# A fused attention and two-layer MLP kernel on one core: the written-out orders of VectorE and ScalarE set anew, and six output tiles held back at the end

## The reference

```python
# q, k, v: 4 batches, 8 heads, 576 positions, head size 64, float32
pooled = softmax(mean4(q) @ mean4(k).T / 8) @ mean4(v)      # 144 positions, repeated 4 times
local  = softmax(where(|i - j| < 4, q @ k.T / 8, -1e9)) @ v
x = (repeat(pooled, 4) + local)                             # -> [2304 tokens, 512]
x = (sigmoid(x @ w_gate) * (x @ w_val)) @ w_out             # 512 -> 1536 -> 512
h = x @ w_in2;  out = (h * sigmoid(1.702 * h)) @ w_out2     # 512 -> 2048 -> 512
```

## Time and profile before

| | before |
|---|---|
| median of the runs | 888.92 us |
| profiled execution, its own time | 887.71 us |
| its span, first to last instruction | 886.0 us |
| TensorE busy, matmul | 863.6 us (97%) |
| VectorE busy | 639.4 us (72%) |
| GpSimd busy | 591.5 us (67%) |
| ScalarE busy | 486.2 us (55%) |
| granted TensorE clock | 1.00 over the whole span |
| DMA, mean | 208 GB/s |

### The profile page before, as it was taken

The page is one execution under the profiler, slowest core; times in us unless marked ns, Lnnn a source line. Parts: engine busy times, 40 slices in busy tenths (PEclk is TensorE's granted clock), DMA queues, the critical chain, the costliest instruction groups (busy, mean ns, idle before and its releaser), DMA issues.

```text
span 886.0 us, 18369 instructions
## 1 busy us (share of the span) xinstructions
PE 863.6 (97%) x6638; PEld 830.4 (94%) x6638; DVE 639.4 (72%) x1140; ACT 486.2 (55%) x1083; POOL 591.5 (67%) x471
## 2 busy tenths in 40 slices
PE   8999999999999999999999899999999999999997
PEld 6877899999999999899999899999999999999996
DVE  5767545555658575967575977878787878878777
ACT  5777754545436355545355555664566456555651
POOL 5688988988658639773639765864678645845541
PEclk9999999999999999999999999999999999999999
DMA  8877366686956796828596815425236750646422
GB/s 323 264 229 215 136 255 243 224 341 259 355 163 221 258 351 225 298 80 286 204 338 234 275 47 191 156 95 202 96 119 214 286 190 25 213 171 225 160 75 72
DMA packets 74778, 184.26 MB, mean 208 GB/s; under 512 B 5569, under 2 KB 31169, under 8 KB 71873
## 3 DMA queue, kind: packets, MB, share of 16 engines
q1 hardware_dynamic: 74688, 183.10, 59.0%
HBM read 141.66 MB, written 41.42 MB: 207 GB/s over the span
## 4 chain that ended last, share of the span: by engine, by line
PE 81%; issue 6%; DVE 5%; POOL 4%; ACT 2%; DMA 1%; SPq 1%; DVEq 0%; ACTq 0%; POOLq 0%
PE o_ps L788 9%; PE o_ps L790 9%; PE o_ps L789 9%; PE d_ps L642 6%; PE o_ps L633 6%; PE d_ps L644 5%; PE d_ps L643 5%; PE s_ps L642 5%; PE s_ps L644 5%; PE s_ps L643 5%; PE t_ps L642 3%; PE t_ps L644 3%; PE t_ps L643 3%; PE o_ps L606 1%; POOL v L2099 1%
## 5 line engine op out<-in xcount | busy, mean ns | idle before, releaser
L788 PE MATMUL o_ps<-g_hi,v 128*128 128x384 f32 x504 | 169.7, 337 | 5.4 <-DVE att L1752 2.7
L790 PE MATMUL o_ps<-g_hi,v 128*128 128x384 f32 x504 | 169.6, 337 | 0.0
L789 PE MATMUL o_ps<-g_lo,v 128*128 128x384 f32 x504 | 169.4, 336 | 0.0
L1752 DVE TENSOR_TENSOR att<-o_ps,att 128x384 f32<-128x384 f32 x212 | 117.2, 556 | 55.7 <-PE o_ps L790 54.3
L2099 POOL TENSOR_TENSOR v<-v_f,v 128x512 fp32r<-128x512 f32 x72 | 95.3, 1343 | 51.4 <-ACT v L1055 51.4
L642 PE MATMUL d_ps<-xs_hi,w 128*128 128x384 f32 x360 | 122.3, 340 | 5.9 <-DVE s_ps L1610 3.4
L2099 POOL TENSOR_TENSOR v<-raw,v 128x512 fp32r<-128x512 f32 x54 | 71.1, 1316 | 82.9 <-ACT v L1048 82.9
L644 PE MATMUL d_ps<-xs_hi,w 128*128 128x384 f32 x360 | 120.7, 335 | 0.0
L643 PE MATMUL d_ps<-xs_lo,w 128*128 128x384 f32 x360 | 120.6, 335 | 0.0
L642 PE MATMUL s_ps<-xs_hi,w 128*128 128x384 f32 x300 | 101.9, 340 | 2.8 <-POOL xs_lo L2129 2.3
L788 PEld LDWEIGHTS o_ps<-g_hi,v 128*128 128x128 f32 x504 | 94.7, 188 | 7.2 <-issue 4.2
(11 more groups left out here) (181 smaller groups left out, 2122.0 us busy)
## 6 DMA issues: line engine op xcount, KB each, us to landing
w<-w_split SPq DMA_DIRECT2D x48, 768.0 KB, 7.0
w<-w_split SPq DMA_DIRECT2D x48, 512.0 KB, 7.8
w<-w_split SPq DMA_DIRECT2D x96, 256.0 KB, 5.0
w_split<-w SPq DMA_DIRECT2D x12, 1792.0 KB, 6.8
raw<-in_w_out_dram SPq DMA_DIRECT2D x36, 512.0 KB, 4.5
w_split<-job_w SPq DMA_DIRECT2D x8, 1792.0 KB, 9.5
vw<-in_v_win_dram SPq DMA_DIRECT2D x16, 390.0 KB, 4.8
raw<-in_w_gate_val_dram SPq DMA_DIRECT2D x12, 512.0 KB, 3.9
```

The costliest lines, as they stand in the source:

```text
L788: pe.matmul(bank, vh, gh, start=(start and k == c), stop=False, skip_group_check=True)
L789: pe.matmul(bank, vh, gl, start=False, stop=False, skip_group_check=True)
L790: mm = pe.matmul(bank, vl, gh, start=False, stop=(k == c + 1), skip_group_check=True)
L1752: vec.tensor_tensor(part, value, part, ALU.add).then_inc(y_added, 1)
```

## The change

VectorE's and ScalarE's lists in the four functions are set anew: instructions move by a few places, none is added or dropped. On SP, one load moves behind a store and a load. On TensorE, six tiles of the pair before the last are held back instead of four, `second_pair(38, 4)` to `(38, 6)`. All saved gated values of the last two groups get places of their own in the ring of x (`end`), and gelu no longer waits there for the tiles that read `g_f`. GpSimd's list is as it was.

```diff
...
         job_w = {i: place(f"job_w{i}", [P, 2, NP, WG], F32R, at=at_x(i)) for i in (7, 4, 1)}
         job_f = {i: place(f"job_f{i}", [P, 2, NP, WG], at=at_x(i)) for i in (7, 4, 1)}
         job_raw = {i: place(f"job_raw{i}", [P, 4, WG], at=at_x(i) + 8 * NP * WG) for i in (7, 4, 1)}
-        end_11 = place("end_11", [P, NT], at=at_x(4))
-        end_21 = [place(f"end_21{i}", [P, NT], at=at_x(2 + i)) for i in range(2)]
+        end = place("end", [P, 2, 3, NT], at=at_x(2))
...
             return att[:, p, c * PASS + t * NT:c * PASS + (t + 1) * NT]
         def saved_11_at(k):
-            return g_f[k % 2][:, 0, T2, :] if k != NG - 2 else end_11[:, :]
+            return g_f[k % 2][:, 0, T2, :] if k < NG - 2 else end[:, k % 2, 0, :]
         def saved_12_at(k):
-            return g_f[k % 2][:, 1, T2, :]
+            return g_f[k % 2][:, 1, T2, :] if k < NG - 2 else end[:, k % 2, 1, :]
         def saved_21_at(k):
-            return g_f[k % 2][:, 0, T4, :] if k < NG - 2 else end_21[k % 2][:, :]
+            return g_f[k % 2][:, 0, T4, :] if k < NG - 2 else end[:, k % 2, 2, :]
         def gated_at(k, n, bank):
...
             for k in range(G1 - 1):
                 if k >= 1 and k + 1 < G1:
                     load_out(k + 1)
-                load_in(LAST[k + 1] + 2)
                 if k == 2:
                     store_job(0)
                     load_job(1)
+                load_in(LAST[k + 1] + 2)
                 if k == 4:
                     store_job(1)
                 if k < G1 - 2:
...
                 p3(FIRST[c])
                 head(FIRST[c + 1])
                 step(FIRST[c + 2])
-                for i in range(NP if c + 4 < NG else NP - 2):
+                for i in range(NP if c + 4 < NG else NP - 3):
                     second_pair(c, i)
             c = NG - 2
             p4(FIRST[c])
             p3(FIRST[c])
             head(FIRST[c + 1])
-            second_pair(c - 2, NP - 2)
+            second_pair(c - 2, NP - 3)
             p3(FIRST[c + 1])
             p4(FIRST[c + 1])
+            second_pair(c - 2, NP - 2)
             second_pair(c - 2, NP - 1)
             for i in range(NP):
                 second_pair(c, i)
...
                 sigmoid(k, 12, z_bank)
             def gelu(k, n, bank):
-                if n in SLOT and (n != 21 or k < NG - 2) and (n != 11 or k != NG - 2):
+                if n in SLOT and k < NG - 2:
                     act.wait_ge(y_ready, g_free(k, SLOT[n]))
                 nc.scalar.activation(gated_at(k, n, bank), bank[FIRST[k] % 2], ACT.Gelu_apprx_sigmoid).then_inc(gated[n], 1)
...
                 n, m = FIRST[k + 1], LAST[k + 1]
                 snap_p1(n)
                 hi22(k)
-                hi21(k)
                 if k == 5:
                     round_t1(1)
-                sig11(k + 1)
                 if k == 5:
                     round_t3(1)
+                sig11(k + 1)
+                hi21(k)
                 snap_u2(n)
                 hi12(k)
+                snap_u3(n)
                 if m < MADE:
                     round_in(m)
                     round_in_sums(m)
-                snap_u3(n)
                 if k == 5:
                     round_t4(1)
                     round_b22(1)
...
                 if k in (1, 3):
                     job_a(k // 2)
                     job_s(k // 2)
+                sig12(k + 1)
+                snap_p1(m)
                 if k == 4:
                     round_b11(1)
                     round_b21(1)
-                sig12(k + 1)
-                snap_p1(m)
                 if FIRST[k + 2] < MADE:
                     round_in(FIRST[k + 2])
                 snap_u2(m)
-                hi11(k + 1)
                 if FIRST[k + 2] < MADE:
                     round_in_sums(FIRST[k + 2])
+                hi11(k + 1)
                 snap_u3(m)
                 if k == 4:
                     round_t2(1)
...
                 if last:
                     round_b11(q + 1)
                 snap_u2(FIRST[d])
+                if c in (G1 + 2, G1 + 6, G1 + 8):
+                    job_a({2: 3, 6: 5, 8: 6}[c - G1])
                 hi_t1(c)
                 sig11(d)
+                if last:
+                    round_b21(q + 1)
                 if c == G1:
                     v_s1(c)
                 snap_u3(FIRST[d])
                 hi_t3(c)
-                if c in (G1 + 2, G1 + 6, G1 + 8):
-                    job_a({2: 3, 6: 5, 8: 6}[c - G1])
                 snap_p1(LAST[d])
                 hi_t2(c)
-                if last:
-                    round_b21(q + 1)
                 sig22(d)
                 sig21(d)
                 hi_t4(c)
...
                 if c == G1:
                     job_a(2)
                 snap_u3(LAST[d])
+                snap_p1(FIRST[n])
                 if last:
                     round_t1(q + 1)
-                snap_p1(FIRST[n])
                 hi22(d)
                 if last:
                     round_t3(q + 1)
                 hi21(d)
+                snap_u2(FIRST[n])
+                hi_t1(d)
+                hi_t3(d)
                 if c == G1:
                     job_s(2)
-                snap_u2(FIRST[n])
-                hi_t1(d)
-                snap_u3(FIRST[n])
-                hi_t3(d)
                 hi_t2(d)
                 v_a12(n)
                 hi_t4(d)
                 if last:
                     round_t4(q + 1)
                     round_b22(q + 1)
+                snap_u3(FIRST[n])
                 if c in (G1 + 2, G1 + 8):
                     job_a({2: 4, 8: 7}[c - G1])
-                v_a11(n)
                 if c in (G1 + 2, G1 + 8):
                     job_s({2: 4, 8: 7}[c - G1])
+                v_a11(n)
                 if layer(n) == 1:
                     sig11(n)
                     sig22(n)
...
                 if not late:
                     v_s2(c)
                     v_s4(c)
-                gelu11(d)
                 snap_u2(FIRST[d])
                 hi_t1(c)
                 hi_t3(c)
+                gelu11(d)
                 hi11(d)
                 snap_u3(FIRST[d])
                 hi_t2(c)
+                snap_p1(FIRST[n])
                 if last:
                     round_t1(q + 1)
                 elif late:
...
                 else:
                     v_s3(c)
                     v_a22(c)
-                snap_p1(FIRST[n])
-                hi_t4(c)
                 if last:
                     round_t3(q + 1)
                 gelu22(d)
+                hi_t4(c)
                 gelu21(d)
+                hi21(d)
                 if last:
                     snap_u2(FIRST[n])
-                hi21(d)
                 gelu12(d)
                 if not last:
                     snap_u2(FIRST[n])
...
                 hi_t2(d)
                 if not late:
                     v_a12(n)
+                if first and q + 1 < len(PHASES):
+                    round_b11(q + 1)
+                    round_b21(q + 1)
                 if c == START[q] + 2 and q + 1 < len(PHASES):
                     round_t2(q + 1)
                 hi_t4(d)
-                if first and q + 1 < len(PHASES):
-                    round_b11(q + 1)
-                    round_b21(q + 1)
                 gelu11(n)
                 if last:
                     round_t4(q + 1)
                     round_b22(q + 1)
                 if late:
                     v_a12(n)
+                hi11(n)
                 v_a11(n)
-                hi11(n)
                 gelu22(n)
                 hi22(n)
...
                 d = c + 1
                 gelu21(c)
                 hi21(c)
+                snap_p1(FIRST[d])
                 gelu12(c)
-                snap_p1(FIRST[d])
+                hi_t1(c)
+                snap_u2(FIRST[d])
                 v_s1(c)
-                v_s2(c)
-                v_s4(c)
                 gelu11(d)
-                snap_u2(FIRST[d])
-                hi_t1(c)
                 hi11(d)
                 snap_u3(FIRST[d])
                 gelu22(d)
-                hi_t3(c)
-                v_s3(c)
+                hi22(d)
+                v_s2(c)
                 gelu12(d)
-                hi_t2(c)
                 gelu21(d)
                 hi21(d)
-                hi22(d)
+                v_s4(c)
+                hi_t1(d)
+                hi_t3(c)
+                hi_t3(d)
+                hi_t2(c)
+                hi_t2(d)
+                v_s3(c)
+                hi_t4(c)
                 v_a22(c)
-                hi_t1(d)
-                hi_t4(c)
-                hi_t3(d)
-                hi_t2(d)
                 hi_t4(d)
             act.wait_ge(zeroed, 1)
...
                     low11(c)
                     c22(LAST[c])
                 gate22(c)
+                low22(c)
                 gate21(c)
                 c12(LAST[c])
                 gate12(c)
-                low22(c)
                 make_t1(c)
                 c11(FIRST[d])
                 make_t3(c)
...
```

(59 more changed lines are left out.)

## The result

The changed kernel takes 872.29 us (median of 5 runs, 871.56 to 873.14) against 888.92 (886.49 to 890.87): ratio 0.9821, 95% interval 0.9808 to 0.9834. Forecast were 878.9 and a range of 873.5 to 885.5.

The account below looks back on a forecast made before the run. TensorE's stream was taken to bound the kernel, with only its holes to win. Terms summed to 12.5 us, less 2.5 for new waits: 887.71 - 10.0 = 877.7, plus 1.2 to the median: 878.9; range 873.5 to 885.5.

Parts of the forecast that it names:

- deduction: Over the 18 pairs: 2.5 us taken off the summed gain for some ten new small waits of 0.25 us.
- f: First pair of the next second-layer pass, twice: c22 ahead of low11 removes a wait; 1.5 us gain (0.5 to 2.0).
- Term b: First-layer pairs: low22(c) ahead of gate21(c), job_s(2) behind a snapshot; 0.8 us gain (-0.5 to 1.1).
- a: Entry into the second pass: round_t1 and round_t3 earlier, so GpSimd's chain starts sooner; 0.9 us gain (0 to 1.2).
- c: Ends of first-layer passes, twice: low21(d) earlier, round_t1 later so x_t3 can start first; 3.0 us gain (0 to 4.6).
- Term g: The kernel's end: six tiles held back and values kept apart, p4 of the last pair earlier; 3.3 us gain (1.5 to 4.3).
- e: Last pair of a second-layer pass, twice: x_t3 and round_t3 earlier; 1.2 us gain (-0.6 to 1.9).
- Term d: Second-layer pairs: c22 ahead of low_t2 and low11, gelu11 and hi11 behind hi_t3; 1.8 us gain (-2 to 2.6).
- more: Rival: x_t3 starts first at both passes, no new waits; 872.7 us, 873.9 as a median; chance 0.15.
- Only the end and f: Rival: elsewhere small waits only change places, meeting GpSimd anew; 882.9 us, 884.1 as a median; chance 0.17.
- The slower one: Rival: in layer one's first pass a circle of waits costs five blocks 2.5 us each; median 891.4; chance 0.05.
- such a circle: Layer one, first pass: TensorE's p7, snapshot, round_in, low_in, low_in_sums, TensorE's p6; if closed, 12.5 us lost in all.

Follow-up runs that it names:

- the end with c22: Kernel before with six tiles held back at the end and c22 ahead of low11 in the second layer's pairs: 881.77 us, ratio 0.9929.
- pair_of_one alone: Kernel before with only pair_of_one's two instruction lists (first layer's pairs) set anew: 882.49 us, ratio 0.9923.

## Why the prediction was wrong

The reading of the profile held: only TensorE's holes could be won, and the terms are all there with their sign. The miss is 6.6 us, in these steps.

**The deduction failed: "I take off 2.5, some ten new ones of 0.25".** The new waits did come, and in about that size: followed product by product, TensorE loses 0.1 to 0.4 us at nine places in the trace of the change, 2.6 in all (two of them, 0.32 each, f had counted with 0.25). One of them:

```profile
356.57 0.41 PE L641 MATMUL s_ps<-xs_hi,w 128*128 128x384 f32 x1 [0.18 <-ACT snap L1104]
```

But what went is 18.6 us, where the terms had 12.5, and among it are small waits of before that no term had named, such as those at p7 at 318.25, 408.82 and 452.90 us (0.25 each). With all new waits in them the terms measure 16.1. Waits that come may be taken off only against those that go unnamed.

**Term b was mis-sized, 0.8 for 2.02.** Some 1.7 of it are six small waits, 0.1 to 0.6 us each. The largest, 0.62 with what follows from it, is the snapshot behind job_s, which the term had named:

```profile
281.44 0.45 PE L642 MATMUL s_ps<-xs_hi,w 128*128 128x384 f32 x1 [0.34 <-ACT snap L1098]
```

The two at 267.84 and 273.51 go with low22's move alone (0.33 in that trace); the three at p7 were in no term. Another 0.15 is the difference of two larger steps that the forecast had at nothing: the 0.76 lost and the 0.91 won at make_t1's two places. As much lies at the borders to a and c. I cost low22's move at the hole that it fills and did not ask what starts behind it. Had make_t1 been free at both places in the profile of before, as it was in that of the end with c22, b would have measured about 0.5; so a part of this miss is the luck of one profile. The evidence stood in the earlier trace rows, 0.553 to 2.268 with a median of 0.56; I used it for a rival only.

**Term g, 3.3 for 4.25; e, 1.2 for 1.92; c, 3.0 for 3.74.** In g I left 1.7 us of waits; the trace has 0.17 at p3:

```profile
838.02 0.41 PE L641 MATMUL d_ps<-xs_hi,w 128*128 128x384 f32 x1 [0.17 <-DVE s_ps L1610]
```

and two holes after it, at 850.86 and 853.35, of under 0.3 between starts. In e, x_t3 ran 0.95 us at both places (613.70 and 731.76) instead of 1.63, which the term did not have; no run takes e apart. In c I took a mean of the case in which x_t3 stays long and the one in which it does not. It started 0.75 ahead of GpSimd's T1 at both ends and ran 0.95, my estimate being 1.0. The Trainium skill's rule in full (SBUF — State Buffer, "SBUF: two separate sides": the shared port pair as an exclusive lock, first come first served) gave 3.8, the trace 3.74, and with round_t1 early x_t3 ran 2.36. The rule should have been the forecast. Term d (1.8 for 2.09) and f (1.5 for 1.38) were about right.

**Term a came in part as I had it, 0.73 for 0.9.** TensorE is 1.05 to 1.08 us later in this trace when it gets here, so my 237.9 for GpSimd's T1 is about 239.0 on its clock; it started at 238.88, and T3 followed without its wait. But T1 met x_t3, which was first, and took 2.41 instead of 1.84:

```profile
238.07 1.52 DVE L1721 TENSOR_TENSOR xs_sum<-att 128x768 f32<-128x768 f32 x1
...
238.88 2.41 POOL L2132 TENSOR_TENSOR xs_lo<-xs_sum,xs_hi 128x768 fp32r<-128x768 f32 x1
```

So the chain is 0.6 earlier by that trace's own measure and not 1.0. TensorE won it at two small steps ahead of p3, and the wait at p3 is still 0.49 (251.52), where I had it going. 0.2 of the 0.73 stands ahead of all this, at 130 us.

**From profile to median.** I put 1.2 us on top, as in the kernel before. The gain between first product and last matmul is 16.13, between the medians 16.63; 0.5 stays unassigned. It is no more than the starts scatter, and the falls of the clock are in the median of before and not in its profile.

So 2.5 (deduction) + 3.6 (terms) + 0.5 = 6.6. Of the rivals the one with "more", 873.9 at a chance of 0.15, came nearest. Half of its mechanism held, x_t3 first at both ends; the other half, no new waits, did not, so its number is in part luck. "Only the end and f" falls: pair_of_one alone brings 0.77%. The slower one did not come. That such a circle exists is shown, but that closing it cost 12.7 us where the prediction had 12.5 is luck: it was closed by another move, at p1, nine times 1.2 us and 1.6 more, and not five times 2.5 at p6.

## What to carry to other kernels

Where two engines share a port, look in the profile of before for pairs that start within a tenth of a microsecond, and for groups whose longest is four times their median: an edit that puts VectorE's clearly first is worth most of the difference. Which of the two an edit puts first has to be walked: low22 alone put make_t1 first, the whole change put it second. Walk new orders with the waits that come inside the walk, and take off nothing more for them afterwards. When a kernel is bound by one engine, compare two executions from that engine's first changed instruction to its last, and look at the granted clock of both. Start times in two traces can only be compared once the delay between them at that point is taken off.

## What was not expected of the hardware

A VectorE instruction with both inputs in SBUF that is recorded as starting 0.04 or 0.05 us ahead of GpSimd's runs in 0.56 us, and GpSimd's takes 2.21; recorded 0.01 ahead it waits for GpSimd (1.84) and takes 2.27. That is so at all ten places in the five traces of kernels in which pair_of_one has its old order: five starts 0.04 or 0.05 ahead ran free, five starts 0.01 to 0.03 ahead were late. One at a time, first come first served, fits both; below 0.04 us the recorded starts don't say who was first.

In five traces TensorE's granted clock fell from 1.00 to 0.50 at or 1.2 us behind the end of a wait of 1.25 or 2.3 us, and matmuls then started 0.32 us apart instead of 0.17; it cost 1.5 us in three of them. The same waits stand in other traces without it.
